# Joining the token mixer's input on GpSimd, and two super-units under way at once, in a WKV, mixer and gated-convolution kernel

## The reference

```python
for t in range(S):                    # S = 768, per batch (4) and head (8), D = 48
    cur = einsum('bhd,bhe->bhde', u[None] * kt, vt)
    y[:, :, t] = einsum('bhd,bhde->bhe', rt, state + cur)
    state = wt[:, :, :, None] * state + einsum('bhd,bhe->bhde', kt, vt)
```

```python
h  = maximum(x^T @ w_tok1, 0) @ w_tok2;  u  = x + h^T      # 768 -> 256 -> 768 tokens
h2 = maximum(u @ w_ch1, 0) @ w_ch2;      x2 = u + h2       # 384 -> 1536 -> 384 channels
```

## Time and profile before

| what | value |
|---|---|
| median of 3 runs | 673.71 us (673.36 to 677.86) |
| the profiled execution | 673.79 us |
| its span, first to last instruction | 671.6 us |
| TensorE busy | 620.4 us, 92% of the span |
| VectorE busy | 392.1 us, 58% |
| ScalarE busy | 177.6 us, 26% |
| GpSimd busy | 96.7 us, 14% |
| TensorE's mean granted clock, share of full | 0.987 |

### The profile page before, as it was taken

One profiled execution on the slowest core, in us unless ns is written; L12 is line 12 of the kernel. 1 busy time (PEld: TensorE's weight loads), 2 busy tenths in 40 slices (PEclk: granted clock), 3 DMA queues, 4 the chain that ended last, 5 costly groups with the idle time before them and its releaser, 6 DMA issues.

```text
span 671.6 us, 24044 instructions
## 1 busy us (share of the span) xinstructions
PE 620.4 (92%) x11188; PEld 597.3 (89%) x11188; DVE 392.1 (58%) x609; ACT 177.6 (26%) x306; POOL 96.7 (14%) x110
## 2 busy tenths in 40 slices
PE   2588589999998999999998999999999999999995
PEld 2588589999998999999998999999999999999994
DVE  4895485494768284475768285376766252352615
ACT  2203324223232132113223132213223132221313
POOL 2214633303003000303003000403002000000000
PEclk9999789999999999999999999999999999999998
DMA  9811552400301200210400300120000000000000
GB/s 243 247 51 52 164 157 80 120 8 10 124 4 43 89 1 27 70 41 3 107 26 11 122 1 26 38 73 3 2 26 2 24 11 14 1 1 25 2 24 23
DMA packets 13331, 35.27 MB, mean 53 GB/s; under 512 B 1584, under 2 KB 7984, under 8 KB 11888
## 3 DMA queue, kind: packets, MB, share of 16 engines
q1 hardware_dynamic: 9776, 29.01, 15.2%
q10 hardware_dynamic: 3456, 4.72, 2.0%
HBM read 29.01 MB, written 4.72 MB: 50 GB/s over the span
## 4 chain that ended last, share of the span: by engine, by line
PE 80%; DVE 10%; issue 3%; ACT 2%; DMA 2%; POOL 1%; SPq 0%; DVEq 0%; ACTq 0%; POOLq 0%
PE ps L697 80%; DVE gate L670 3%; DMA w<-in_w_dram 2%; DVE rk L539 1%; DVE at L594 1%; DVE hid L619 1%; DVE rk_next L539 1%; DVE wp L539 1%; ACT x2s L429 1%; DVE us L632 1%; POOL st L412 1%; POOL st L415 1%; DVE xf L647 0%; DVE xf L651 0%; ACT gate L429 0%
## 5 line engine op out<-in xcount | busy, mean ns | idle before, releaser
L697 PE MATMUL ps<-us,ch 128*128 128x256 f32 x1296 | 167.1, 283 | 1.4 <-DVE us L632 0.8
L697 PE MATMUL ps<-hid,ch 128*128 128x256 f32 x1296 | 166.8, 283 | 0.0
L697 PEld LDWEIGHTS ps<-us,ch 128*128 128x128 f32 x1296 | 157.1, 188 | 4.8 <-DVE us L632 2.0
L697 PEld LDWEIGHTS ps<-hid,ch 128*128 128x128 f32 x1296 | 157.2, 188 | 1.5
L619 DVE SCALAR_TENSOR_TENSOR hid<-ps,hid 128x512 fp32r<-128x512 f32 x72 | 49.8, 691 | 136.5 <-ACT hid L488 136.5
L488 ACT ACTIVATE hid<-ps 128x512 fp32r<-128x512 f32 x72 | 42.8, 596 | 154.8 <-PE ps L697 154.8
L594 DVE COPY_PREDICATED at<-masks,ps 128x512 f32<-128x512 uint8 (+1 forms) x72 | 65.3, 911 | 23.8 <-PE ps L697 23.8
L670 DVE SCALAR_TENSOR_TENSOR gate<-xf,cw,gate 128x256 f32<-128x256 f32 x144 | 73.2, 556 | 2.9 <-ACT gate L504 2.0
L697 PE MATMUL ps<-rk 48*64 48x32 f32 x2240 | 52.3, 251 | 10.9 <-issue 8.4
L697 PEld LDWEIGHTS ps<-rk 48*64 48x64 f32 x2240 | 48.9, 171 | 15.0 <-issue 13.0
L412 POOL TENSOR_TENSOR st<-st,wp 112x192 f32<-112x192 f32 x40 | 24.8, 621 | 210.0 <-ACT ds L429 202.7
(11 more groups left out here) (72 smaller groups left out, 614.6 us busy)
## 6 DMA issues: line engine op xcount, KB each, us to landing
rk<-in_rk_dram SPq DMA_DIRECT2D x7, 896.0 KB, 6.0
vs<-in_v_dram SPq DMA_DIRECT2D x12, 384.0 KB, 7.2
out_dram<-gate ACTq DMA_DIRECT2D x24, 192.0 KB, 3.3
...
```

Of the source, the lines that this page charges most:

```text
L697: return nc.tensor.matmul(out, lhsT, rhs, start=start, stop=stop, skip_group_check=True, **kw)
```

## The change

Four things, in the words of the code:

- **x is joined.** GpSimd adds `xs[:, HI]` and `xs[:, LO]` into `x_sum` by `join_x`, 2 units (128x768 elements) at a time, three times a batch. `x_sum` lies where `xs[:, HI]` lies, so a join waits until the batch's last G1 product has read x. U then transposes `x_sum`, one transpose where HI and LO took two, and does the two channel blocks of a bank first and their transposes after them.
- **A twice.** `at_next` stands beside `at` for every other super-unit (by `landing` instead of `home`), and takes the room of `w_next`; the decays w of a super-unit are now loaded (`load_w`) once those of the one before have been used.
- **k is turned in k's place**: `kt` is written over k, so that `fk` is free when L1 has read it. F waits for L1 of the super-unit before.
- **New order** in the prologue and at three places of the trip; a memset of unused PSUM columns and one of `at_next` at the start.

```diff
 PROLOGUE = """
     F:0 W:0 L1:0 F:1 W:1 w:0 L2:0 L1:1 w:1 L2:1 L4:0 F:2 L4:1 W:2 L8:0 L8:1 L16:0 L1:2 L2:2 w:2 w:3 L4:2 L32:0
-    L8:2 L16:1 L16:2 w:4 T:0 L32:1 w:5 D:0 L32:2 T:1 T:2 D:1 w:6 A:0 B:0 A:1 w:7 Z:0 w:8 P:0 D:2 B:1 Z:1 F:3 w:9
-    w:10 W:3 A:2 L1:3 B:2 Z:2 P:1 w:11 L2:3 w:12 L4:3 P:2 G1.0.0 G1.0.1 w:13
+    L8:2 w:4 T:0 L16:1 L16:2 L32:1 w:5 D:0 L32:2 T:1 T:2 D:1 w:6 A:0 B:0 A:1 w:7 Z:0 w:8 P:0 F:3 D:2 B:1 Z:1 w:9
+    L1:3 w:10 W:3 A:2 L2:3 B:2 Z:2 P:1 w:11 w:12 L4:3 P:2 G1.0.0 G1.0.1 w:13
 """
...
     L8:0 U.0.0 L16:0 C1.0.0 L32:0 w:14 C1.0.1 T:0 w:15 w:16 C2.0.0 D:0 F:1 C1.0.2 W:1 C2.0.1 C1.0.3 w:17 C2.0.2
-    A:0 L1:1 B:0 Z:0 C2.0.3 C1.0.4 C1.0.5 L2:1 C2.0.4 w:18 w:19 L4:1 C2.0.5 X.0.0 L8:1 U.1.0 L16:1 C1.1.0
-    tap.0.0 L32:1 C2.1.0 T:1 tap.0.1 C1.1.1 tap.0.2 D:1 C1.1.2 gate.0.0 tap.0.3 V.0.0 A:1 C2.1.1 M.0.0 B:1 Z:1
-    tap.0.4 gate.0.1 F:2 S.0.0 C2.1.2 M.0.1 W:2 S.0.1 C1.1.3 L1:2 C1.1.4 L2:2 C2.1.3 L4:2 O.0.0 L8:2 C1.1.5
+    A:0 L1:1 B:0 Z:0 C2.0.3 C1.0.4 L2:1 C1.0.5 w:18 w:19 L4:1 C2.0.4 C2.0.5 X.0.0 L8:1 U.1.0 L16:1 C1.1.0
+    tap.0.0 L32:1 C2.1.0 T:1 tap.0.1 C1.1.1 tap.0.2 D:1 C1.1.2 gate.0.0 tap.0.3 V.0.0 A:1 M.0.0 C2.1.1 B:1 Z:1
+    tap.0.4 gate.0.1 F:2 S.0.0 C2.1.2 M.0.1 W:2 S.0.1 C1.1.3 C1.1.4 L1:2 L2:2 C2.1.3 L4:2 O.0.0 L8:2 C1.1.5
...
-        rk_next, w_next = sb("rk_next", [P, 2 * PH * CH]), sb("w_next", [P, PH * CH])
+        rk_next, at_next = sb("rk_next", [P, 2 * PH * CH]), sb("at_next", [P, PH * CH])
...
+        with ExitStack() as joined:
+            x_sum = joined.enter_context(nc.sbuf_tensor("x_sum", [P, UNITS, DM], F32))
         xs = sb("xs", [P, 2, UNITS, DM], F32R)
...
-        at_sides = [at[:, :].rearrange("p (h t) -> p h t", h=PH) for _, _, _, at, _ in homes]
+        at_sides = [at[:, :].rearrange("p (h t) -> p h t", h=PH)
+                    for at in (homes[0][3], at_next, homes[1][3], homes[2][3])]
...
-        kt_sides = [fk[:, 0:PH * D].rearrange("p (h d) -> p h d", d=D) for fk in first_rk]
+        kt_sides = [k[:, 0:PH * D].rearrange("p (h d) -> p h d", d=D) for k in k_sides]
...
-            def load_rkw(s):
+            def load_rk(s):
 
                 b, i = divmod(s, SUPERS)
                 at, before = landing(s), landed_before(s)
                 if before is not None:
                     sp.wait_ge(y_done, 4 * (before + 1))
-                    sp.wait_ge(kt_done, 4 * (before + 1))
-                    sp.wait_ge(next_done[1], before + 1)
+                    sp.wait_ge(ds_done, 4 * (before + 1))
                 sp.dma_start(rk_sides[at][0:RD, :], rk[b, i]).then_inc(rk_in[at], 16)
-                sp.dma_start(w_sides[at][0:RD, :], w[b, i]).then_inc(decay_in[at], 16)
+
+            def load_w(s):
+
+                b, i = divmod(s, SUPERS)
+                need(sp, next_done[1], tenant(s))
+                need(sp, decay_done[2], tenant(s))
+                sp.dma_start(w_sides[home(s)][0:RD, :], w[b, i]).then_inc(decay_in[home(s)], 16)
...
                 if kind == "weight" and n + 2 < NW:
                     load_weight(n + 2)
+                elif kind == "att" and name == "W" and (n == 1 or 3 <= n < NS - 1):
+                    load_w(max(n + 1, SUPERS))
                 elif kind == "att" and name == "B":
                     if n == 1:
-                        load_rkw(4)
+                        load_rk(4)
                     elif 3 <= n < NS - 2:
-                        load_rkw(n + 2)
+                        load_rk(n + 2)
...
-                need(pool, ds_done, 4 * tenant(s))
+                need(pool, lev_done[1], 4 * tenant(s))
...
+            def join_x(b, j):
+
+                need(pool, mm_done, ring_filled(RING_USE[(b, "G1", 0, 1)]))
+                units = slice(2 * j, 2 * j + 2)
+                nc.gpsimd.tensor_tensor(x_sum[:, units, :], xs[:, HI, units, :].bitcast(F32),
+                                        xs[:, LO, units, :].bitcast(F32), ALU.add).then_inc(x_joined, 1)
+
...
+                elif kind == "dense" and name == ("G1", 0, 1):
+                    join_x(n, 0)
+                elif kind == "dense" and name == ("U", 0, 0):
+                    join_x(n, 1)
+                    join_x(n, 2)
...
 
-                bank = bank_of(s, name)
-                if name == "L1":
-                    dve.wait_ge(lev_done[1], 4 * (s + 1))
-                    if s == 0:
-                        dve.wait_ge(mask_in, 16)
-                        dve.wait_ge(zero_done, ZEROS)
-                    need(dve, y_done, 4 * tenant(s))
-                    out = at_sides[home(s)].rearrange("p (w h) t -> p w (h t)", w=2)
+                bank, m = bank_of(s, name), int(name[1:])
+                dve.wait_ge(lev_done[m], 4 * (s + 1))
+                if s == 0:
+                    dve.wait_ge(mask_in, 16)
+                if INTO[(s, name)]:
+                    dve.wait_ge(into_done[landing(s)], INTO[(s, name)])
+                else:
+                    dve.wait_ge(zero_done, ZEROS)
+                if landed_before(s) is not None:
+                    dve.wait_ge(y_done, 4 * (landed_before(s) + 1))
+                if m == 1:
...
-                    .then_inc(into_done[name], 1)
+                    .then_inc(into_done[landing(s)], 1)
...
+            nc.vector.memset(ps[:, PAIR_BANK[2]:, CH // 2 * PH // 2:PH // 2 * D], 0.0).then_inc(zero_done, 1)
             for side in at_sides:
                 nc.vector.memset(side, 0.0).then_inc(zero_done, 1)
...
                 elif kind == "U":
                     ready = RING_USE[(b, "G1", 0, 1)]
                     need(pe, ring_free[ready % 2], ring_read(ready))
-                    for dt in range(DT):
-                        if dt == 2:
-                            use = RING_USE[(b, "U", j, 1)]
+                    for n, dts in enumerate((range(2), range(2, DT))):
+                        use = RING_USE[(b, "U", j, n)]
+                        if n:
                             need(pe, ring_free[use % 2], ring_read(use - 2))
-                        bank = ps[:, RING + use % 2, dt % 2 * TT:(dt % 2 + 1) * TT]
-                        rows = (lambda a, kt: h1[:, a, kt, dt * P:(dt + 1) * P],
-                                lambda a, kt: wcols("tok2", a, kt * S + j * TT, TT))
-                        hi_terms(bank, range(FT // P), *rows, True, True)
-                        lo_terms(bank, range(FT // P), *rows, True, False)
-                        for sc in range(2):
-                            for part in (HI, LO):
-                                ins = mm(bank[:, sc * P:(sc + 1) * P],
-                                         xs[:, part, 2 * j + sc, dt * P:(dt + 1) * P].bitcast(F32), ident[:, :],
-                                         False, is_transpose=True)
-                        if dt:
-                            ins.then_inc(mm_done, 1)
+                        banks = {dt: ps[:, RING + use % 2, dt % 2 * TT:(dt % 2 + 1) * TT] for dt in dts}
+                        for dt in dts:
+                            rows = (lambda a, kt: h1[:, a, kt, dt * P:(dt + 1) * P],
+                                    lambda a, kt: wcols("tok2", a, kt * S + j * TT, TT))
+                            hi_terms(banks[dt], range(FT // P), *rows, True, dt == dts[0])
+                            lo_terms(banks[dt], range(FT // P), *rows, True, False)
+                        need(pe, x_joined, since(b, TILES, j + 1))
+                        for dt in dts:
+                            for sc in range(2):
+                                ins = mm(banks[dt][:, sc * P:(sc + 1) * P], x_sum[:, 2 * j + sc, dt * P:(dt + 1) * P],
+                                         ident[:, :], False, is_transpose=True)
+                        ins.then_inc(mm_done, 1)
                 elif kind == "C1":
```

More of the change, by code:

```diff
@@ L44 @@
 SLOTS = 2 * QS + 1
-ZEROS = 3
+ZEROS = 5
 MASK = PH // 2 * CH // 2
@@ L158, in landings @@
     return 1 if s < 4 else s // 2 if s % 2 == 0 else (s - 1) // 2
+INTO = {}
+for _kind, _n, _s in PROGRAM:
+    if _kind == "att" and _s[0] == "L":
+        INTO[(_n, _s)] = sum(landing(n) == landing(_n) for n, _ in INTO)
 TOK1_CHUNKS = 2
@@ L240, in build @@
         rk_sides = [homes[0][0], rk_next, homes[1][0], homes[2][0]]
-        w_sides = [homes[0][1], w_next, homes[1][1], homes[2][1]]
+        w_sides = [w for _, w, _, _, _ in homes]
         r_sides = [rk[:, 0:PH * CH] for rk in rk_sides]
@@ L254, in decays @@
             if m == 1:
-                return w_sides[landing(s)][0:RD, :]
+                return w_sides[home(s)][0:RD, :]
             return wp_sides[home(s)][0:RD, W_AT[m]:W_AT[m] + PH * CH // m]
         rk_in = [sem(f"rk_in{i}") for i in range(4)]
-        decay_in = [sem(f"decay_in{i}") for i in range(4)]
+        decay_in = [sem(f"decay_in{i}") for i in range(3)]
         v_in = [sem(f"v_in{i}") for i in range(2)]
@@ L268, in build @@
         next_done = {m: sem(f"next_done{m}") for m in LEVELS}
```

(23 more changed lines are left out.)

14 lines of the change are left out of this document (8 added, 6 removed).

## The result

The changed kernel takes **681.09 us**, the median of 10 runs (676.04 to 683.54); the kernel before took 673.18 beside it (10 runs, 670.91 to 677.86). The ratio is 1.0104, 95% interval 1.0078 to 1.0130: 1% slower. 682.4 was forecast. The profiled execution is the quickest of the ten, 676.04 us around a span of 674.2, so its trace shows less of the loss than the median has.

What follows compares the result with a forecast made beforehand. TensorE was taken as the bound, busy 620.4 of 671.6 us, with a chain through all engines in the first 100 us. Sum: 673.8 - 7.8 - 1 - 3 + 14.9 + 1 + 4.5 = 682.4 us; own range 674 to 691.

Steps and rivals of the forecast that it cites:

- 1. The transposes: In U, 72 of 144 transposes go, 0.109 us each on TensorE's own path: -7.8 us.
- 2. A twice and the freed `fk`: Six waits of L1's masked copy for TensorE's B step fall away in the three trips: -1 us, ends 0 and 2.
- 3. The prologue: L1:3 runs while TensorE waits for GpSimd's states and its old place closes up: -3 us, ends +3 and -7.
- 4. The joins: GpSimd joins behind G1.0.1 take turns with VectorE's taps, M starts 5.0 us late: +14.9 us for three trips; batch 0 +1.
- all of it would stand before `O.2.0`: At a trip's end, TensorE has no slack, so the 5 us delay comes out as idle time at O.2.0.
- a sign that the forecast is wrong: At the trips' ends: if O.2.0 waits under 1 us, the forecast is wrong and the time is near 662.
- 5. The clock: Behind the joins' waits TensorE falls to 1.2 GHz, 1.5 us at each of three trip ends: +4.5 us, ends 0 and 8.7.
- hidden joins: Rival: joins and taps pass each other, so only terms 1 to 3 stay: 662.0 us; chance 18%.
- one join in three: Rival: joins 2 and 3 start only in VectorE's gaps, a trip's end costs 1.83 us: 668.5 us; chance 12%.
- a starved prologue: Rival: SyncE's new order brings weights 2 and 3 so late that term 3 turns to +3: 688.4 us; chance 5%.
- a clock that stays low for longer, with a held first trip: Rival: longer low clock adds 4.2 us and the held first trip 3: 689.6 us; chance 10%.

## Why the prediction was right

**1. The transposes, -7.8 us: right.** 8.2 us between the two runs without joins, 7.5 by their ratios. The four of a piece are still 0.11 us apart:

```profile
99.20 0.60 PE L737 MATMUL ps<-ident,x_sum 128*128 128x128 f32 x4
```

The Trainium skill (TensorE: Matmul & The Clock Gate, "Wait — 56ns, not 53.3ns?") has 55.6 ns for 128 columns and would have made the term 4.0 us; trace and runs have twice that for these float32 transposes. TensorE never waited for `x_sum` in the changed kernel, as foreseen.

**2. A twice and the freed `fk`, -1 us: within its ends, the reason wrong.** Six waits of the masked copies were to fall away. Six are left, of 3.8 us at most instead of 5.3, 17.3 us in all instead of 23.8, and the time doesn't show it: 1.0104 against 1.0090 with one `A`.

**3. The prologue, -3 us: the place right, the size too large.** `L1:3` (the first line) runs in the time in which TensorE waited for the states, but the two waits behind it took most of it back, as the text had allowed for:

```profile
77.33 1.13 PE L737 MATMUL ps<-fk 48*64 48x64 f32 x64
82.09 0.95 PE L737 MATMUL ps<-vs,at 64*64 64x48 f32 x32 [3.64 <-POOL st L436]
82.75 1.14 PE L737 MATMUL ps<-st,rk 48*64 48x48 f32 x32
85.55 1.93 PE L737 MATMUL ps<-rk_next 48*64 48x32 f32 x64 [1.65 <-DVE rk_next L572]
```

The first trip's first product of `U` starts at 97.7 instead of 98.9: 1.2 us. Together with term 2 it was to be 4 us, and the change without joins gives 2.2 (the ratio of 0.9967; 0.8 to 3.6 by its interval). New orders of the trips also gave something that the prediction had not priced, which the run with the old orders hints at; how the 2.2 us divide among trips and prologue is left open.

**4. The joins, +14.9 us and +1: the mechanism right, the size a little large.** `M` came 4.24 us later in trip 1, and 4.98 were computed, so 12.7 instead of 14.9 for three. The three taps show the difference: 1.83, 1.83 and 1.33 us each were computed as the time that they are held, and over their 0.48 us they lasted 1.5, 1.6 and 1.1 longer. What failed is the sentence that all of it would stand before `O.2.0`: two thirds stood before the third bank of `V.2.0`, and in trip 1 `O.2.0` had no wait at all, which the text had called a sign that the forecast is wrong and the time near 662. The sum did not suffer, since it is one chain. Batch 0's joins cost 0.6 us at the first `C1` (a wait of 0.82 us for `us`, and 0.25 in the run with the high part alone), against 1.

```profile
102.62 2.38 PE L737 MATMUL ps<-us,ch 128*128 128x256 f32 x18 [0.82 <-DVE us L670]
```

**5. The clock, +4.5 us: right in kind, uneven in detail.** 1.5 us for each of three trips was forecast; the profiled run has 1.9 and 1.5 in two of them and none in the third, 3.4 in all. Other profiles with these joins have 4.8 to 6.0; with one `A`, `O.2.0` lasted over 4.6 us in all three trips. So 4.5 is in their midst, and how often the clock falls was not foreseen but averaged.

**The sum.** Joins and clock were put at 20.4 us and cost 18.3; transposes, `A` and prologue at -11.8 and gave 673.18 - 662.81 = 10.4. The two errors are of opposite sign, +2.1 and -1.4; with the base, 673.8 in the sum and 673.2 by the median, that leaves the 1.3 us between 682.4 and 681.1. By ratios the parts are 16.8 and 9.8, and the errors 3.6 and 2.0. That they cancel in part is luck; the direction does not hang on it, since 16.8 to 18.3 lost against 9.8 to 10.4 gained is slower either way. Its own range was summed wrongly: the ends of terms 3 to 5 give 673 to 697 and not 674 to 691, which changes nothing here. **The rivals:** hidden joins are refuted by taps of 2.0 us; one join in three by three taps held in every trip; a starved prologue by a first `U` that came earlier; a clock that stays low for longer, with a held first trip, by 3.4 to 6.0 us of clock where it needed 8.7, and 0.6 us in the first trip where it needed 4.
